# The last two blocks of a first feed-forward layer, moved into the second layer's groups of 15 block products

## The reference

```python
state = f[:, :, t, :, None] * state + einsum('bhd,bhe->bhde', k[:, :, t], v[:, :, t])   # f = sigmoid(f_logit)
y[:, :, t] = einsum('bhd,bhde->bhe', q[:, :, t], state)
x = y.transpose(0, 2, 1, 3).reshape(3072, 384)
x = ((x @ w_a) * (x @ w_b)) @ w_out                      # first FFN, inner width 1536
p = domain_probs / domain_probs.sum(-1)                  # four experts, every token uses all
out = sum(p[:, e:e+1] * (maximum(x @ w1[e], 0) @ w2[e]) for e in range(4))   # second FFN, inner width 1024 each
```

## Time and profile before

| what | value |
|---|---|
| median of 3 runs | 1312.23 us (1311.81 to 1313.07) |
| span of the profiled execution | 1310.4 us; no time outside the span is given for it, the median of the runs is 1.8 us above |
| PE, PEld busy | 99%, 98% |
| DVE, ACT, POOL busy | 63%, 47%, 42% |
| chain that ended last | PE 97% |
| granted TensorE clock | 1.000 |
| attention beside the first FFN | until about 380 us |
| first FFN alone | about 380 to 560 us |
| second FFN | about 560 to 1307 us, 17.2 us for a full group |

### The profile page before, as it was taken

The page is one execution under the profiler, slowest core; times in us unless marked ns, Lnnn a source line. Parts: engine busy times, 40 slices in busy tenths (PEclk is TensorE's granted clock), DMA queues, the critical chain, the costliest instruction groups (busy, mean ns, idle before and its releaser), DMA issues.

```text
span 1310.4 us, 23459 instructions
## 1 busy us (share of the span) xinstructions
PE 1301.5 (99%) x8223; PEld 1278.5 (98%) x8223; DVE 825.4 (63%) x1678; ACT 622.0 (47%) x1259; POOL 549.4 (42%) x560
## 2 busy tenths in 40 slices
PE   8999999999999999999999999999999999999998
PEld 7999999999999999999999999999999999999998
DVE  7855554555433324367777777777677776777765
ACT  7654544444432323354545554545544455544442
POOL 3321211212135856234445644446544447444441
PEclk9999999999999999999999999999999999999999
DMA  8512122122204343132332343322343313343211
GB/s 253 157 59 60 54 62 60 53 62 61 62 1 144 99 140 125 31 97 80 96 97 72 91 136 91 89 91 69 107 125 96 95 63 93 98 131 98 87 60 49
DMA packets 71686, 117.59 MB, mean 90 GB/s; under 512 B 7120, under 2 KB 49808, under 8 KB 71568
## 3 DMA queue, kind: packets, MB, share of 16 engines
q1 hardware_dynamic: 71568, 116.08, 29.4%
HBM read 102.94 MB, written 14.55 MB: 90 GB/s over the span
## 4 chain that ended last, share of the span: by engine, by line
PE 97%; DVE 1%; DMA 1%; SPq 0%; issue 0%; ACT 0%; DVEq 0%
PE bank L1885 12%; PE bank L1887 11%; PE bank L1886 11%; PE bank L2119 10%; PE bank L2120 10%; PE bank L2121 10%; PE bank L2013 8%; PE bank L2015 8%; PE bank L2014 8%; PE bank L1829 2%; PE bank L1880 2%; PE bank L1868 1%; PE bank L2091 1%; PE bank L2090 1%; PE bank L2089 1%; PE bank L1812 1%
## 5 line engine op out<-in xcount | busy, mean ns | idle before, releaser
L1270 POOL TENSOR_TENSOR wu<-w_r,wu 128x640 fp32r<-128x640 f32 (+1 forms) x132 | 200.6, 1522 | 315.1 <-ACT wu L954 315.1
L2119 PE MATMUL bank<-wd,h_hi 128*128 128x384 f32 x768 | 259.8, 338 | 0.5 <-issue 0.3
L2120 PE MATMUL bank<-wd,h_hi 128*128 128x384 f32 x768 | 257.6, 335 | 0.0
L2121 PE MATMUL bank<-wd,h_lo 128*128 128x384 f32 x768 | 257.1, 335 | 0.0
L1678 DVE SCALAR_TENSOR_TENSOR xt<-bank,pn,xt 128x384 f32<-128x384 f32 x288 | 177.2, 615 | 101.0 <-PE bank L2121 91.7
L981 ACT ACTIVATE h_hi<-h 128x384 fp32r<-128x384 f32 x240 | 124.6, 524 | 193.4 <-DVE h L1628 81.5
L2015 PE MATMUL bank<-x_lo,wu 128*128 128x384 f32 x600 | 202.6, 338 | 0.0
L2013 PE MATMUL bank<-x_hi,wu 128*128 128x384 f32 x600 | 201.4, 336 | 0.0
L2014 PE MATMUL bank<-x_hi,wu 128*128 128x384 f32 x600 | 200.8, 335 | 0.0
L1885 PE MATMUL bank<-xs_hi,wab 128*128 128x384 f32 x570 | 196.8, 345 | 1.4 <-ACT a_sb L992 1.4
L1886 PE MATMUL bank<-xs_hi,wab 128*128 128x384 f32 x570 | 191.2, 335 | 0.0
(11 more groups left out here) (158 smaller groups left out, 2406.2 us busy)
## 6 DMA issues: line engine op xcount, KB each, us to landing
w_r<-weight_sums SPq DMA_DIRECT2D x120, 320.0 KB, 2.9
raw<-w SPq DMA_DIRECT2D x48, 576.0 KB, 3.9
unit<-fkq SPq DMA_DIRECT2D x28, 504.0 KB, 4.2
v_in<-v_chunks SPq DMA_DIRECT2D x32, 144.0 KB, 3.9
out<-xt SPq DMA_DIRECT2D x24, 192.0 KB, 4.4
weight_sums<-w_s SPq DMA_DIRECT2D x10, 384.0 KB, 4.4
weight_sums<-w SPq DMA_DIRECT2D x40, 64.0 KB, 2.7
raw<-w SPq DMA_DIRECT2D x6, 384.0 KB, 3.2
```

What stands on the lines that cost most here:

```text
L1270: eng.tensor_tensor(wu_piece(g, n, 1), wu_raw(g, n), wu_piece(g, n, 0).bitcast(f32), ALU.subtract).then_inc(s_ulo, 1)
L2119: eng.matmul(o, hh, w_hi, start=(f == fs[0]), stop=False)
L2120: eng.matmul(o, hh, w_lo, start=False, stop=False)
L2121: mm = eng.matmul(o, hl, w_hi, start=False, stop=(f == fs[-1]))
```

## The change

Only six blocks of the first FFN (`PLAIN` = 6) keep the old loop, which has 214 steps now. The last two blocks are a pass of their own, in the form of the second FFN's groups: 8 groups, in turns one of three tiles of a (15 products into `h2`) and one of the same three tiles of b (15 products into `hb`). VectorE multiplies the two in the b group (`product`); in the kernel before the product of a and b stands on VectorE as well (L1445), so GpSimd loses no work. The split of the result is `h1_round` and `h1_rest`, and the six output tiles stand three in the next a group and three in the next b group. They are added into `xt` transposed as before (`weigh`, `acc_1`). The passes are then: first FFN blocks 6 and 7, second FFN blocks 0 and 1, 2 and 3, 4 and 5, 6 and 7. In each pass of the second FFN the short group comes first instead of last.

The weight sums are now made for 18 groups (8 of w_a and w_b, 10 of w1), from step 31 at a pace of 9, beside the attention, with one buffer `w_s` in place of two, so the next sums wait until the last are stored. The x sums of the first pass are made at steps 184 to 204.

```diff
-    N1 = NB1 * FT1
+    PLAIN = 6
+    N1 = PLAIN * FT1
...
+    PASSES = [(1, b) for b in range(PLAIN // 2, NP)] + [(2, b) for b in range(NP)]
+    GROUPS = [(p, q) for p, (ffn, _) in enumerate(PASSES) for q in (range(2 * NF) if ffn == 1 else (NQ, *range(NQ)))]
...
-    SUMS_AT, SUMS_PACE = CMIN_AT, 8
+    SUMS_AT, SUMS_PACE = 31, 9
...
     def x2_at(n):
-        return SUMS_AT + 4 + 8 * n if n < 8 else 3 * FT1 * (NB1 - 1) + 2 + 2 * (n - 8)
+        return CMIN_AT + 9 + 2 * n
...
             def w_sum(q, n):
                 if n == 0:
                     eng.wait_ge(s_wr, w_loads(q))
-                    eng.wait_ge(s_wst[q % 2], W_STORED * (q // 2)) if q >= 2 else eng.wait_ge(s_y, NU)
+                    if q:
+                        sums_stored(eng, q - 1)
...
+            def h1_round(g, n):
+                o = H_ORDER[n]
+                eng.wait_ge(s_mul, products(g) + n + 1)
+                h2_free(g)
+                eng.activation(h2_hi[:, half(g), o, :], hb[:, o, :], ACT.Copy).then_inc(s_h2hi, 1)
...
+            def product(g, n):
+                o = H_ORDER[n]
+                eng.wait_ge(s_add, adds(g) + (3, 6, 7, 8, 9, 10)[n])
+                eng.tensor_tensor(hb[:, o, :], h2[:, o, :], hb[:, o, :], ALU.mult).then_inc(s_mul, 1)
+
+            def h1_rest(g, n):
+                o = H_ORDER[n]
+                eng.wait_ge(s_h2hi, results(g) + n + 1)
+                eng.tensor_tensor(h2_lo[:, half(g), o, :], hb[:, o, :], h2_hi[:, half(g), o, :].bitcast(f32),
+                                  ALU.subtract).then_inc(s_h2lo, 1)
...
             def weigh(g, n):
...
+                if ffn(g) == 1:
+                    d, to = tile_bank(g, n), acc_1(g, n)
...
+                    if q_of(g) == 1:
+                        eng.tensor_copy(to, d).then_inc(s_acc, 1)
+                    else:
+                        eng.wait_ge(s_acc, tiles(g - 2) + n + 1)
+                        eng.tensor_tensor(to, to, d, ALU.add).then_inc(s_acc, 1)
...
+                elif ffn(g) == 1:
+                    add(g, 1)
+                    add(g, 2)
+                    add(g, 3)
+                    product(g, 0)
+                    if q > 1:
+                        weigh(g - 2, 3)
+                    h1_rest(g, 0)
+                    add(g, 4)
+                    if nxt:
+                        plain_lo(nxt, 2)
...
-                    if g:
-                        down_2(g - 1, n)
-                    elif n == 4:
-                        down_1(N1 - 1)
+                    if g == 0:
+                        if n == 4:
+                            down_1(N1 - 1)
+                    elif ffn(g) == 2:
+                        down(g - 1, n)
+                    elif makes_a(g):
+                        if n % 2 == 0:
+                            down(g - 1, n // 2)
+                    elif q_of(g) > 1:
+                        if n % 2 == 1:
+                            down(g - 2, 3 + n // 2)
```

More of the change, by code:

```diff
@@ L487, in f_tiles, with makes_a, makes_h, full @@
+        def makes_a(g):
+            return ffn(g) == 1 and q_of(g) % 2 == 0
+        def makes_h(g):
+            return not makes_a(g)
+        def full(g):
+            return ffn(g) == 1 or q_of(g) < NQ
+        def sums_of(g):
+            return q_of(g) if ffn(g) == 1 else 2 * NF + q_of(g)
         def f_tiles(q):
             return range(FG * q, FG * q + (FG if q < NQ else LAST))
-        def shares(g):
-            fs = f_tiles(g % GP)
+        def fs_of(g):
+            return range(FG) if ffn(g) == 1 else range(len(f_tiles(q_of(g))))
@@ L505, in results, with products, parts @@
+        def products(g):
+            return sum(2 * FG if ffn(x) == 1 and makes_h(x) else 0 for x in range(g))
         def results(g):
-            return sum(2 * len(f_tiles(x % GP)) for x in range(g))
+            return sum(2 * len(fs_of(x)) for x in range(g) if makes_h(x))
+        def parts(g):
+            return len(shares(q_of(g))) if ffn(g) == 2 else 1
         def tiles(g):
-            return sum(TT * len(shares(x)) for x in range(g))
+            return sum(TT * parts(x) for x in range(g) if makes_h(x))
@@ L1671, in weigh @@
                     eng.wait_ge(s_tile, tiles(g) + part + 1)
-                    if q == 0 and i == 0:
+                    if not full(g):
                         eng.tensor_scalar(acc(b, t), d, w, None, ALU.mult).then_inc(s_acc, 1)
                     else:
-                        eng.wait_ge(s_acc, tiles(g) + part if i else
-                                    tiles(g - 1) + len(shares(g - 1)) * (n + 1))
+                        eng.wait_ge(s_acc, tiles(g) + part if i else tiles(g - 1) + parts(g - 1) * (n + 1))
                         eng.scalar_tensor_tensor(out=acc(b, t), in0=d, scalar=w, in1=acc(b, t),
@@ L2101, in down_2 @@
                 if n % 3 == 0:
-                    there = results(g) + ((5, 6) if g % GP < NQ else (2, 4))[n // 3]
+                    there = results(g) + ((5, 6) if full(g) else (2, 4))[n // 3]
                     eng.wait_ge(s_h2hi, there)
@@ L2106, in down_2 @@
                 cols = slice(t % 3 * 128, (t % 3 + 1) * 128)
-                for i, (_, fs) in enumerate(shares(g)):
-                    part = len(shares(g)) * n + i
+                for i in range(parts(g)):
+                    part = parts(g) * n + i
                     if tiles(g) + part >= 2:
```

692 lines of the change are left out of this document (439 added, 253 removed).

## The result

The changed kernel takes 1343.01 us (median of 4 runs, 1341.26 to 1344.04), the kernel before 1312.02 (4 runs): ratio 1.0231, 95% interval 1.0217 to 1.0244. That is 31 us slower where 4.7 were forecast, and outside the range of 1309 to 1324. The profiled execution has a span of 1341.8 us.

A forecast was written before the change was run, and what follows sets the result against it. TensorE, busy 99% of the span, was taken as the bound. Matmuls -12.5, waits +16.1, collisions +1.2, ends +0.5 and -0.6 gave +4.7 us on 1312.2: 1316.9 us, range 1309 to 1324.

The forecast's parts named there:

- Matmuls, -12.5: Last two first-FFN blocks: 576 matmuls instead of 648, 72 fewer at 0.174 us each, -12.5 us.
- Walk of waits, 16.1: First pass, four seams: TensorE waits 5.3, 2.65 twice and 5.5 us, sum 16.1, bounds 13.8 to 19.2; chance 0.5.
- over 90: Sign expected in the first pass: VectorE over 90% busy in the b groups.
- VectorE keeps up: Rival, first pass: results arrive sooner, waits halve to about 8 us, total 1307.6 us, 4.6 us faster; chance 0.14.
- gain and waits cancel: Rival, first pass: waits of 11 to 14 us, total time between 1310 and 1314.5 us; chance 0.18.
- I take 0, at most 0.5 for each of three changes: Three later changes of pass, second FFN: low parts in time by the same walk, so 0 us, at most 0.5 each.
- Collisions, +1.2: b groups: VectorE's two-SBUF-input instructions lengthened beside GpSimd's weight pieces, 1.4 us, 1.2 on the path, between 0 and 4.
- whole collisions: Rival, b groups: each such VectorE instruction waits out half a GpSimd piece, 14 us, 8.5 on path, 1324; chance 0.06.
- Weight sums beside the attention, 0: Attention: GpSimd's extra weight sums just fit nine steps, 17 to 18.4 us a set, costing 0, range 0 to 8.
- The rival that they disturb it: Attention: GpSimd or SyncE falls behind, gates or loads come late, 6 to 10 us more, 1323 to 1327; chance 0.12.
- Ends, -0.1: Last group's down tile waits for low parts, +0.5; group 0's two waits of 0.3 us go, -0.6.
- The reading of the waits before: Kernel before: TensorE's longest waits are 1.4 and 0.3 us, once each; nothing else holds it inside the kernel.

The follow-up runs named there:

- experiment 2: The changed kernel without VectorE's six products of a and b in each of the four b groups, output incomplete; 1324.83 us, ratio 1.0098.
- experiment 5: The kernel of experiment 1 with the same instructions of the first pass in another order on VectorE, ScalarE and TensorE; 1314.94 us, ratio 1.0020.
- experiment 1: The changed kernel with GpSimd making the three w2 low parts before the fifth x sum's low part ahead of later pass changes; 1326.11 us, ratio 1.0102.
- experiment 3: The changed kernel with 24 unused matmuls ahead of the wait for the first down tile at each of four pass changes; 1335.27 us, ratio 1.0181.
- experiment 6: The kernel of experiment 1 with GpSimd's up-weight low parts of groups 2 to 8 made for 8 of each 128 columns; 1322.47 us, ratio 1.0073.
- experiment 8: The kernel of experiment 1 with all weight-sum sets but the first made for 8 of 128 columns; 1325.83 us, ratio 1.0107.
- mended kernel: The kernel of experiment 1: the changed kernel with GpSimd's order altered at the later changes of pass; 1326.11 us.
- experiment 4: The kernel of experiment 1 with all six products of a and b of each b group on GpSimd instead of VectorE; 1325.59 us, ratio 1.0103.

## Why the prediction was wrong

**Matmuls, -12.5: right.** 72 fewer, at the distance of the starts.

**Walk of waits, 16.1: right in kind, 3 short.** 19.1 measured, VectorE's meetings with GpSimd included, in the places named: 1.49 at the tenth product of group 1 for ACT's copy; 1.96 at the third product of group 2 for add 10; 1.5 at the down tiles of groups 4 and 6; 4.85 in group 8, where 3.0 were walked, and 1.7 of the 1.85 between them are two low parts that GpSimd lengthened. VectorE decides most of them (experiment 2), by its order more than by its load: it was busy 86 to 88% in the b groups 3, 5 and 7 (experiment 5), not over 90. "VectorE keeps up" is out, and so is "gain and waits cancel".

**"I take 0, at most 0.5 for each of three changes": this step failed, and it is the largest.** It was 6.0 to 7.2 us each, 19.4 together. The walk followed VectorE and ScalarE into the tenth group and checked that the low parts of relu(h2) were in time; they are late by 0.5 us, within its bound (experiment 1). It gave GpSimd no list there. That list had the w2 pieces behind an instruction that waits for ScalarE. Experiment 1 took it away for 16.9 us. The text of the change was enough to see it: two lists, one semaphore.

**The granted clock, for which the sum has no term: failed.** "Any wait added in TensorE's list lengthens it by its full size", says the prediction; some waits cost more. In the first pass the clock fell behind waits of 1.80 and 0.99 us close together and behind one of 1.35, and it fell at each of the four waits of 4.4 to 4.7 us. The trace of before had a wait of 1.36 us at 31 us, behind which the clock stayed at 1.00, and none of that size in the second FFN, so it could not tell what one does there; both levels of the clock should have been carried as bounds. It cost some 12 us in all, 7.7 of them shown by experiment 3 at the four changes of pass.

**Collisions, +1.2: mis-sized.** The products and low parts of the first pass lasted 692 and 621 ns, 5.1 us more busy time than at 550 ns where 1.4 had been reckoned; the x sums, up to 1942 ns, had been left out altogether. Cutting the weight pieces alone gave 3.6 us (experiment 6). The average of the second FFN's low parts, 0.03 us, was the wrong row: it spreads the few that met GpSimd over the many that did not. The maximum of 1328 ns was the right one, as a size per meeting. The rival "whole collisions" had the mechanism; its 8.5 us on the path are more than the 3.6 that the weight pieces gave, but these are only a part, since GpSimd's other work stayed.
The Trainium skill, page "SBUF — State Buffer", section "Who interferes with whom", says that such a pair excludes each other for the whole instruction. The rows under experiment 6 agree: three VectorE instructions end 0.41 us behind GpSimd's ends, and so do 69 of 70 in the trace of before, within 0.03 us.

**Weight sums beside the attention, 0: right** (experiment 8, -0.3 us with the intervals overlapping). GpSimd was busy 65% there, as reckoned (66%). The rival that they disturb it is out.

**Ends, -0.1: right** within what the rows show: 0.2 us for L1829 at the last group, none in group 0.

**The reading of the waits before: incomplete.** The prediction calls 1.4 and 0.3 us the longest; 1.6, 1.0 and 0.5 us stand there too, in the first 15 us. Nothing in the sum hangs on them.

## What to carry to other kernels

When work is moved to a place where it borders on a new neighbour, follow the lists of all engines there, the one that is half idle too: an in-order list is late by its first blocked instruction, not by its load. An order is a parameter of its own: with the same instructions in another order the same change went from 2.3% slower to 0.35% faster. Where TensorE will wait, count the clock behind the wait as well, and lay GpSimd's long SBUF instructions beside VectorE's PSUM instructions, not beside those with two SBUF inputs.

## What the runs showed of the hardware

- The granted clock fell to its lower level (0.32 us per matmul of 384 columns instead of 0.174) at idle stretches of TensorE in an engine otherwise 97% busy: for 8 to 18 matmuls behind each wait of 4.4 to 5.0 us, and for some 7 behind one of 1.35 us in group 4 of the mended kernel, but not behind the same wait in group 6 of it. Matmuls that nothing uses, put into four such waits, kept it at 1.00 (experiment 3).
- A VectorE instruction with two SBUF inputs took up to 1942 ns instead of 550 when GpSimd was at work, and ended 0.39 to 0.44 us behind GpSimd's instruction in 69 of 70 cases in the kernel before; adds with one input in PSUM stayed at 539 to 559 ns on average in the first pass.
- GpSimd's products of 128x384 took 1138 ns on average, VectorE's 552 to 735. Moved to GpSimd they left the time as it was, with VectorE's low parts beside them up from 620 to 917 ns (experiment 4).
